# Experts 1 to 7 in units of 640 rows, with weights stationary in the first layer

## What is computed

```
logits = x @ w_gate
noisy_logits = logits + log1p(exp(x @ w_noise)) * noise
top2 = argpartition(-noisy_logits, 2, axis=1)[:, :2]
top2_w = softmax over the two
for e in range(E):                       # E = 8
    for k in range(2):
        mask = top2[:, k] == e
        h = maximum(x[mask] @ w1[e], 0)  # 512 to 1024
        out[mask] += top2_w[mask, k, None] * (h @ w2[e])   # 1024 to 512
```

## Time and profile before

| | us |
|---|---|
| median of 3 runs | 1062.14 (1061.77 to 1064.2) |
| profiled execution, its own time | 1058.88 |
| its span in the trace, first to last instruction | 1057.1 |
| mean granted clock of PE, share of full speed | 0.999 |

### The profile page before, as it was taken

How to read it: one execution, slowest core, us unless ns; L and a number is a source line. 1 busy time by engine, 2 the same in 40 slices (tenths; PEclk the granted TensorE clock), 3 DMA queues, 4 the chain that set the end, 5 groups by cost and what they waited for, 6 DMA issues and landing times. The chain is left out here.

```text
span 1057.1 us, 20933 instructions
## 1 busy us (share of the span) xinstructions
PE 1026.6 (97%) x5935; PEld 882.7 (83%) x5936; DVE 584.0 (55%) x1193; ACT 475.3 (45%) x1108; POOL 374.4 (35%) x407
## 2 busy tenths in 40 slices
PE   6989899999999999999999999999999999999997
PEld 5777798889989899899888788888888888888885
DVE  4787756576576676765876734344343434434222
ACT  5988645354534534544456323233332333333221
POOL 2776666122222222221231334334343433335322
PEclk9999999999999999999999999999999999999999
DMA  9988721000000000005025444333233433411221
GB/s 181 207 196 184 234 60 51 31 2 1 29 1 30 1 0 30 1 0 189 2 57 196 146 140 153 135 136 140 103 140 106 160 124 134 146 59 60 66 65 62
DMA packets 100535, 99.34 MB, mean 94 GB/s; under 512 B 72493, under 2 KB 72973, under 8 KB 100496
## 3 DMA queue, kind: packets, MB, share of 16 engines
q1 hardware_dynamic: 89120, 67.16, 22.1%
q0 software_dynamic: 9760, 31.29, 8.6%
q10 hardware_dynamic: 1616, 0.39, 0.2%
HBM read 79.79 MB, written 20.07 MB: 94 GB/s over the span
## 5 line engine op out<-in xcount | busy, mean ns | idle before, releaser
L1478 POOL TENSOR_TENSOR g_lo<-gate,g_hi 128x384 fp32r<-128x384 f32 x95 | 97.5, 1026 | 298.5 <-ACT g_hi L870 298.4
L146 PE MATMUL ps<-x_hi,w_lo 128*128 128x384 f32 x384 | 133.4, 347 | 1.3 <-DVE gate L1053 1.2
L916 ACT ACTIVATE h_hi<-ps 128x512 fp32r<-128x512 f32 x80 | 43.5, 597 | 197.2 <-PE ps L678 197.2
L146 PE MATMUL ps<-w_hi,h_lo 128*128 (+1 forms) x320 | 128.6, 402 | 2.9 <-DVE h_lo L1260 1.7
L146 PE MATMUL ps<-w_hi,xe_lo 128*128 (+1 forms) x320 | 128.9, 403 | 1.2 <-DVE w_lo L1240 0.6
L148 PE MATMUL ps<-x_hi,w_hi 128*128 128x384 f32 x384 | 129.1, 336 | 0.0
L147 PE MATMUL ps<-x_lo,w_hi 128*128 128x384 f32 x384 | 128.7, 335 | 0.0
L148 PE MATMUL ps<-w_hi,xe_hi 128*128 (+1 forms) x320 | 125.3, 392 | 0.0
L148 PE MATMUL ps<-w_hi,h_hi 128*128 (+1 forms) x320 | 125.2, 391 | 0.0
L147 PE MATMUL ps<-w_lo,xe_hi 128*128 (+1 forms) x320 | 124.5, 389 | 0.0
L147 PE MATMUL ps<-w_lo,h_hi 128*128 (+1 forms) x320 | 124.4, 389 | 0.0
(11 more groups left out here) (186 smaller groups left out, 2074.4 us busy)
## 6 DMA issues: line engine op xcount, KB each, us to landing
xT<-in_w SPq DMA_DIRECT2D x32, 1024.0 KB, 5.2
out<-table SPq DMA_DIRECT2D x18, 256.0 KB, 3.2
y_rows<-y_sb SPq DMA_DIRECT2D x6, 768.0 KB, 3.5
w_raw<-in_w_in SPq DMA_DIRECT2D x8, 512.0 KB, 4.8
y_sb<-in_w_out SPq DMA_DIRECT2D x16, 256.0 KB, 2.7
q_raw<-in_q SPq DMA_DIRECT2D x40, 96.0 KB, 3.6
v_raw<-in_v SPq DMA_DIRECT2D x28, 128.0 KB, 3.3
k_raw<-in_k SPq DMA_DIRECT2D x37, 96.0 KB, 3.5
```

The lines of the kernel that those rows point to most:

```text
L146: nc.tensor.matmul(psum, s_lo, m_hi, start=start, stop=False)
L916: nc.scalar.activation(h2[0][:, 4 * i:4 * i + 4, :], eT[:, 4 * i:4 * i + 4, :], ACT.Copy).then_inc(h_hi, 1)
L1478: nc.gpsimd.tensor_tensor(g2[1][:, f % 2, :], gate[:, f % 2, :], g2[0][:, f % 2, :], ALU.subtract).then_inc(glo_done, 1)
```

## The change

Expert 0 stays as it was, in tiles of 128 rows (its last tile number n is now computed by itself, and the engines' loops over tiles end there). Experts 1 to 7 run in units of UB = 5 blocks of 128 rows, each expert in as many units as its rows need, at least one. A unit works in two pieces of 320 rows (UH): block 2 lies half in each. SLOTC becomes 20, so the table has 160 columns.

In a unit's first layer a 128 x 128 block of w1 is stationary and 320 transposed tokens move, so the result comes out with hidden units on the partitions, in eight groups f that alternate between two banks of PSUM. ACT's relu writes the high part straight from there, DVE's `max` and `subtract` the low part; PE begins group f when the low part of group f-2 is done. The transposes of the hidden values (`transpose_h`) and h_row are not needed in a unit. The second layer is as it was, block by block, with three banks in turn. The order on PE:

```diff
+            def unit_first(u, piece, e):
+                if piece == 0:
+                    pe.wait_ge(w_lo, QUANTA * e + 2)
+                pe.wait_ge(u_xlo, 2 * UB_A * u + UB_A * (piece + 1))
+                for f in range(FC2):
+                    pe.wait_ge(u_hlo, 2 * FC2 * u + FC2 * piece + f + 1)
+                    for d in range(DC):
+                        x = split_product(nc, psH[:, f % 2, 0:UH], [w[:, d, f * P:(f + 1) * P] for w in unit_weights(e)[0]],
+                                          [x[:, d, piece_at[piece]] for x in u_x], d == 0, d == DC - 1)
+                    x.then_inc(u_l1, 1)
+            def unit_second(u, piece, e):
+                if piece == 0:
+                    pe.wait_ge(w_lo, QUANTA * e + QUANTA)
+                for j in summed(piece):          # 0, 1 in piece 0; 2, 3, 4 in piece 1
+                    pe.wait_ge(u_done, UB * u + j + 1)
+                    for f in range(FC2):
+                        if j == summed(piece)[0]:
+                            pe.wait_ge(u_hlo, 2 * FC2 * u + FC2 * piece + f + 3)
+                        x = split_product(nc, psO2[j % UB_A], [h[:, f, block_at[j]:block_at[j] + P] for h in u_h],
+                                          [w[:, f, :] for w in unit_weights(e)[1]], f == 0, f == FC2 - 1)
+                    x.then_inc(u_l2, 1)
+            def unit(u, e):
+                unit_first(u, 0, e)
+                unit_x(u, 1)                     # transposes of blocks 3, 4
+                unit_second(u, 0, e)
+                unit_first(u, 1, e)
+                if e < E - 1:
+                    unit_x(u + 1, 0)             # blocks 0, 1, 2 of the next unit
+                unit_second(u, 1, e)
+                if e == E - 1:
+                    unit_x(u + 1, 0)
...
                 transpose_x(g + 1)
                 second_product(g - 1)
                 transpose_h(g)
+            pe.wait_ge(x_lo, last + 2)
+            unit_x(0, 0)
             second_product(last)
+            for e in range(1, E):
+                first_u, end_u = units_of(pe, e)
+                with pe.Fori(first_u, end_u) as u:
+                    unit(u, e)
```

ACT and DVE (the weight parts of the next expert stand in an If that holds in an expert's first unit):

```diff
+            def unit(u, e, first_u):             # ACT
+                unit_h(u, 0)                     # 8 relus of 128 x 320
+                unit_x(u, 1)
+                unit_parts(u, e, first_u, (0, 1))
+                unit_h(u, 1)
+                unit_x(u + 1, 0)
+                unit_parts(u, e, first_u, (2, 3))
...
+            def unit_low_h(u, piece, sent):      # DVE
+                for f in range(FC2):
+                    if piece == 0 and f == 5:
+                        dve.wait_ge(scattered, sent)
+                    dve.wait_ge(u_hhi, 2 * FC2 * u + FC2 * piece + f + 1)
+                    nc.vector.scalar_tensor_tensor(out=u_h[1][:, f, piece_at[piece]], in0=psH[:, f % 2, 0:UH], scalar=0.0,
+                                                   in1=u_h[0][:, f, piece_at[piece]], op0=ALU.max, op1=ALU.subtract
+                                                   ).then_inc(u_hlo, 1)
+            def unit(u, e, first_u, sent):
+                at_col = unit_col(dve, u)
+                unit_low_h(u, 0, sent)
+                unit_low_x(u, 1)
+                unit_weigh(u, 0, at_col)
+                unit_parts(u, e, first_u, (0, 1))
+                for j in summed(0):
+                    unit_finish(u, j)
+                unit_low_h(u, 1, sent)
+                if e < E - 1:
+                    unit_low_x(u + 1, 0)
+                unit_weigh(u, 1, at_col)
+                unit_parts(u, e, first_u, (2, 3))
+                for j in summed(1):
+                    unit_finish(u, j)
+                if e == E - 1:
+                    unit_low_x(u + 1, 0)
...
-                parts(g)
+            unit_low_x(0, 0)
             finish(last)
+            dve.sem_inc(u_hlo, 2)
+            dve.sem_inc(u_done, 2)
```

POOL gathers the sums of a block straight into the buffer in which DVE adds (u_acc, three of them), and scatters from there:

```diff
+            def unit(u):
+                steps = 3 * u + 1
+                at_col, next_col = unit_col(pool, u), unit_col(pool, u + 1)
+                pool.wait_ge(u_read, UB * u + UB_A)
+                unit_x(u, 1, at_col, steps + 1)  # gathers blocks 3, 4
+                nc.gpsimd.tensor_copy(idx_out[:], sidx[:, bass.ds(at_col, UB)]).then_inc(u_ix, 1)
+                pool.wait_ge(u_ix, steps + 2)
+                for j in gathered(0):
+                    unit_sums(u, j)              # sums of blocks 0, 1, 2
+                pool.wait_ge(u_read, UB * u + UB)
+                unit_x(u + 1, 0, next_col, steps + 3)
+                for j in summed(0):
+                    unit_scatter(u, j)
+                    pool.wait_ge(u_sent, 16 * UB * u + 16 * (j + 1))
+                    unit_sums(u, j + UB_A)
+                for j in summed(1):
+                    unit_scatter(u, j)
+                pool.wait_ge(u_sent, 16 * UB * u + 16 * UB)
...
             last = last_tile(pool)
+            pool.wait_ge(w_lo, 2 * QUANTA)
+            unit_x(0, 0, unit_col(pool, 0), 1)
             with pool.Fori(EARLY, last + 1) as g:
```

The tokens of a unit (u_x, u_row) lie in raw where slots 2 and 3 were, so from expert 2 on the weights have two slots. SP waits for the part two before:

```diff
-            with sp.Fori(2, E) as e:
-                load_weights(e)
+            for e in range(2, E):
+                for n in range(QUANTA):
+                    sp.wait_ge(w_lo, QUANTA + n + 1 if e == 2 and n < 2 else QUANTA * e + n - 1)
```

More of the change, by code:

```diff
@@ L139, in build @@
         program(nc, q, k, v, w_in, w_out, w_gate, w_noise, noise, w1, w2, const, at, ident, small, bfc, sm, xT,
[L140 removed]
+                wgt, [a - 4 * WE for a in w_end], raw_at, raw, ybuf, table, slot1, gidx, sidx, plan, x_row, idx_x, out)
 def split_product(nc, psum, stationary, moving, start, stop):
@@ L981, in _ @@
                 expert_tile(g)
+            act.wait_ge(w_lo, 2 * QUANTA)
+            unit_x(0, 0)
+            for e in range(1, E):
+                first_u, end_u = units_of(act, e)
+                with act.Fori(first_u, end_u) as u:
+                    unit(u, e, first_u)
         @block.vector
@@ L1272, in make_plan @@
             def make_plan():
                 link = link_end
-                e_g, done, j_g, left, shift, last, most = (row[:, r, :] for r in range(7))
-                to = left
-                nc.vector.memset(last, 0.0)
-                nc.vector.memset(plan[:, PLAN_FROM, 0:1], QUANTA)
-                n, cum = tiles[:, 0, :], tiles[:, 1, :]
+                e_g, done, j_g, shift = (row[:, r, :] for r in range(4))
+                units, cum, rows, tiles_0 = (tiles[:, r, :] for r in range(4))
@@ L1287, in make_plan @@
-                link(nc.vector.tensor_scalar(n, tiles[:, 3, :], 1.0, None, ALU.max))
-                link(nc.vector.tensor_tensor_scan(cum, sm["one"][0:1, :], n, 0.0, ALU.mult, ALU.add))
-                g = iota[0:1, 0:NG]
+                link(nc.vector.tensor_copy(rows, ps_count[0:1, :]))
+                link(nc.vector.tensor_scalar(units, rows, 1.0 / (UB * P), 0.5 - 0.5 / (UB * P), ALU.mult, ALU.add))
+                link(nc.vector.tensor_scalar(units, units, ROUND, -ROUND, ALU.add, ALU.add))
@@ L1318, in finish_plan @@
-                link(nc.vector.scalar_tensor_tensor(out=done, in0=e_g, scalar=float(QUANTA), in1=most,
-                                                    op0=ALU.mult, op1=ALU.add))
-                link(nc.vector.tensor_scalar(to, done, float(QUANTA), float(E * QUANTA), ALU.add, ALU.min))
-                nc.vector.tensor_copy(plan[:, PLAN_TO, :], to).then_inc(plan_done, 1)
-                nc.vector.tensor_copy(plan[:, PLAN_FROM, 1:NG], to[:, 0:NG - 1]).then_inc(plan_done, 1)
+                e_g, done, j_g, shift = (row[:, r, :] for r in range(4))
@@ new lines, in finish_plan @@
+                units, cum, rows, tiles_0 = (tiles[:, r, :] for r in range(4))
+                u, n = iota[0:1, 0:NG], tiles_0[:, 0:1]
+                link(nc.vector.tensor_tensor(n, rows[:, 0:1], skip[0:1, :], ALU.add))
+                link(nc.vector.tensor_tensor(j_g, u, done, ALU.subtract))
+                link(nc.vector.tensor_scalar(n, n, 1.0 / P, 0.5 - 0.5 / P, ALU.mult, ALU.add))
+                link(nc.vector.tensor_scalar(shift, e_g, float(SLOTC), None, ALU.mult))
+                link(nc.vector.tensor_scalar(n, n, ROUND, -ROUND, ALU.add, ALU.add))
@@ L1432, in _ @@
                 low_h(g)
-                parts(g)
+            unit_low_x(0, 0)
             finish(last)
+            dve.sem_inc(u_hlo, 2)
+            dve.sem_inc(u_done, 2)
+            sent = 16 * last + 16
+            for e in range(1, E):
+                first_u, end_u = units_of(dve, e)
+                with dve.Fori(first_u, end_u) as u:
+                    unit(u, e, first_u, sent)
         @block.gpsimd
@@ L1523, in scatter, with unit_gather, unit_x @@
                                              bounds_check=most, oob_is_err=False).then_inc(scattered, 16)
+            def unit_gather(u, j, idx, c):
+                pool.sem_inc(dma_turn, 1)
```

(16 more changed lines are left out.)

228 lines of the change are left out of this document (153 added, 75 removed).

## The result

| | before | after |
|---|---|---|
| median of 9 runs each, on one chip | 1062.14 us (1060.34 to 1064.69) | 1054.06 us (1051.29 to 1059.4) |
| ratio | | 0.9924, 95% interval 0.9903 to 0.9945 |
| profiled execution: own time, span | 1058.88, 1057.1 us | 1055.48, 1053.7 us |

The change gains 0.76%, 8 us; 21.8 us (2.1%) were forecast. The time lies in the range (1034 to 1056), far from its likeliest value, and that it lies there is luck: the upper end of the range was taken from rivals 1 and 2, and neither of them occurred. By medians 13.7 us are missing (1054.06 against 1040.4). In the profiled execution the end came at 1053.7 where the sum had 1035.3, so 18.4 us are to be found there; this execution took 1.4 us more than its median, that of the kernel before 3.3 less.

A forecast was written before the change was run, and what follows sets the result against it. TensorE (PE), busy 97%, was taken as the bound. Unit 0's start 625.4 + units 405.3 - 1.3 + 0.2 = 1029.6, plus 5.7 gives end 1035.3, as a median 1040.4 us (2.1% gain); range 1034 to 1056.

The forecast's parts named there:

- rival 1: Two-bank handoff binds: ACT and DVE path 0.5 us longer makes PE wait in 112 groups; 14 us, 1054; chance 0.10.
- rival 2: POOL late with gathers of blocks 3, 4: PE stands 1.4 us in each unit; 10 us, 1050; chance 0.07.
- A unit on PE: PE work per five-block unit of experts 1 to 7: 57.9 us, so seven take 405.3 against 429.5 before.
- rival 3: Weight loads of 320-column matmuls can't come closer than 0.174 us: 36 us more, 1077, slower than before; chance 0.06.
- 120 matmuls of 512 columns at 0.2277 = 27.3 us, as before: A unit's second layer on PE: 27.3 us, with the 512-column pitch unchanged.
- The handoff: ACT relu and DVE subtraction between PE's first-layer groups: path 3.27 us against 3.53, covered by 0.26 us.
- Weights, POOL and DVE at the seams of units: Weight conversion, gathers of blocks 3, 4 and DVE's finishes between units: all covered, cost 0; gathers by 1.3 to 1.9 us.
- The drain between expert 0 and unit 0: PE idles 2.2 us for gathers, then 2.5 us for the finish; unit 0 starts at 625.4; bounds 0 and 9 us.
- the shorter plan: The plan loses some 0.4 us of DVE steps and the table grows to 160 columns: within 0.5 us, taken as 0.
- now 5.7: From PE's end to the span's end: 6.2 us before, 0.5 of it waiting for sums, so 5.7 after.
- Up to the seam: Stretch up to tile 4's transposes, last tile of expert 0: forecast at 612.89 us as before, change 0.
- Rival 4: An expert above 640 rows takes two units: 58 us more, 1098; chance 0.02.

The follow-up runs named there:

- place: Changed kernel plus two unused tiles (192 and 224 bytes), so weights, x_hi and uh_hi begin at residue 64 as in the kernel before: 1048.6 us, ratio 0.9884.
- place_same: Changed kernel plus one 224-byte unused tile behind idx_x, so weights, x_hi and uh_hi all begin at residue 128; executed once, 512-column pitch 227 ns.
- before_apart: Kernel before plus an unused 32-byte tile behind idx_x, so x_hi begins at residue 96 and weights stay at 64: 1070.49 us, ratio 1.0101.
- drains: Changed kernel plus a POOL drain in every unit, ahead of the scatters of its last three blocks: 1044.11 us, ratio 0.9863.
- one_drain: Changed kernel plus a POOL drain in the fourth of the seven units alone; executed once for its profile, closing drain 3.982 us.
- again: Changed kernel measured once more with nothing altered: 1051.25 us beside 1059.14 for the kernel before, ratio 0.993.

## Why the prediction was wrong, point by point

- *A unit on PE.* The 320-column pitch was right: 146.5 ns measured, 147 taken, from a straight line through 384 and 512 columns. So rival 3 (loads too close) fell: loads recorded as 188 ns follow each other at 147 here. The Trainium skill, page "TensorE: Matmul & The Clock Gate", section "Back-to-back issue gap", gives 136 ns for 320 columns as the gap of a matmul by itself, and for a stream of weight loads and matmuls about 131 ns at 512 columns. The trace agrees with neither: 46 steps of 146.5 at 320, and 227 at best at 512. The Trainium skill, page "Perfetto Trace Analysis", section "Identifying the Most-Contended Engine", judges how near PE is to its limit by the busy share of the loads, beside the share of peak arithmetic. By an estimate from that, 332 loads of 188 ns, a unit would take 62.4 us; it took 58.4.
- *The failed step, part one: "120 matmuls of 512 columns at 0.2277 = 27.3 us, as before".* 120 x 0.0056 = 0.7 us more a unit, 4.7 us in seven; in expert 0 place was 0.6 us shorter. The row was read correctly; that a row of an unchanged matmul carries over was the assumption. It depends on where its operands lie, which place_same and before_apart show. The rest of the units' sum was 1.5 us too high, so only 3.2 of it is seen.
- *The handoff* (rival 1): cover of 0.26 us was enough. PE never waits for it in 112 groups. Both durations were right to 0.01 us.
- *Weights, POOL and DVE at the seams of units* (rival 2): cost 0 as taken; no wait for a gather in any unit.
- *The drain between expert 0 and unit 0:* mechanism right, size off: 15.6 us in place of 12.5. Two idle stretches were forecast, 2.2 us for gathers and 2.5 us for the finish. The first came as 4.0 us, because POOL's copy of 2.35 us (0.19 before) and its gather of 2.27 us, some 19 us earlier, made the last two parts of weights late. The prediction had the shorter plan down as a change of under 0.5 us, taken as 0; it didn't have this. The clock then fell, which the text had as a bound of 3 us, a price that no row of the kernel before shows. Here the first seven matmuls of tile 4's second layer took 3.1 us, 1.5 more than at 233 ns, and that filled most of the second idle stretch, of which 0.4 us was left.
- *The failed step, part two, and the largest: "now 5.7" from PE's end to the span's end.* It was 14.1. The term was taken over from the kernel before as a constant, though 1 us of it was a drain whose length depends on what was issued. drains and one_drain show it. The rows of the kernel before show a drain of 0.97 us behind 122 transfers and so give no hint of 8.9, but the term had no bounds either, and it should have had some, as this change replaces most of POOL's transfers. The other 0.5 us of the 8.4 is the wait for sums that the forecast took off: from PE's end to the drain's start it is 5.0 us, as before.
- *Up to the seam:* 3.7 us in the first profile, 0 in that of again; 0 was taken. It is an attention that ended 4.9 us late, 0.7 us in the dense layer, and 2.0 us that expert 0 won, which the sum didn't have. The attention's cause is open.
- *Rival 4* didn't occur.

Of the 18.4 us, the drain's 7.9 and the pitch's 5.1 in the units are shown by removing them; the seam's 3.1 is seen in the timeline and only in part removed; the attention's 4.9 is unexplained. These come to more than 18.4, as the rest of the units' sum and expert 0 came out shorter than forecast.

## What to carry to other kernels

A change that alters the size of a small table moves all tiles behind it. Before a stage is judged, compare the pitch of its unchanged matmuls with the former one; where it has grown, try an unused tile that puts the stationary tile and the moving one at the same residue modulo 256 bytes, and measure. In this kernel that won in the experts and nothing clear in the dense layer. A kernel's last microseconds are a term like any other: look at the instructions of the line that closes the program, and if POOL has issued many indirect DMAs, give it a drain at a point where it is idle anyway. And a transfer whose start hangs on POOL has to be timed with POOL's operations at their slowest beside DVE, not at their median.

## What the runs showed that was not expected

- In the experts, a 512-column matmul of fp32r (the 32-bit type of the operands) follows its predecessor by 227 ns when the stationary tile and the moving weights begin at the same residue modulo 256 bytes, and by 229 to 234 ns in the six other placements. In the dense layer the same residue gave 230.9 ns, and others 230.2 to 234.2. 32 unused bytes made the kernel before 1.0% slower. Matmuls of 320 columns stood at 147 ns throughout, but always with weights and `ux_hi` at the same residue. Why the places matter isn't shown.
- POOL's drain takes 82 ns for each gather or scatter of the units issued since the last drain (3, 48, 105 and 108 of them). The kernel before had 122 and paid for about 12, and expert 0's 17 in the changed one leave nothing that is seen; why is open.
- An attention without a changed line ended 0.9 to 6.6 us later in every profile of the changed program and its variants than in the two profiles of the kernel before; with 32 unused bytes that kernel's own ended 1.0 us later.
- A copy of one column on POOL took 0.19 us in the 3 profiles of the kernel before and its variant, and 2.35 us in all 17 of the changed program, with DVE's subtraction of 2048 columns beginning 0.02 to 0.04 us behind its start in each.
